# The second MLP's first product, taken for two token tiles at once as seven half-size products instead of eight

## The reference

```
h = x @ w_in                                  # (1536, 512) @ (512, 2048)
x2 = (h * 1/(1 + exp(-1.702 h))) @ w_out      # (1536, 2048) @ (2048, 512)
```

```
h = x2 @ w_in                                 # (1536, 512) @ (512, 1024)
e = exp(h - max(h)); sm = e / sum(e); solu = h * sm          # along a token's 1024 values
ln = (solu - mean) / sqrt(var + 1e-6) * g_ln
out = ln @ w_out                              # (1536, 1024) @ (1024, 512)
```

## Time and profile before

| | us |
|---|---|
| median of 3 runs | 672.72 (672.15 to 673.79) |
| profiled execution, its own time | 672.1 |
| its span, first to last instruction | 670.3 |
| PE busy | 639.0 (95%) |
| DVE busy | 434.5 (65%) |
| POOL busy | 419.7 (63%) |
| ACT busy | 321.0 (48%) |

### The profile page before, as it was taken

The page is one execution under the profiler, slowest core; times in us unless marked ns, Lnnn a source line. Parts: engine busy times, 40 slices in busy tenths (PEclk is TensorE's granted clock), DMA queues, the critical chain, the costliest instruction groups (busy, mean ns, idle before and its releaser), DMA issues.

```text
span 670.3 us, 11572 instructions
## 1 busy us (share of the span) xinstructions
PE 639.0 (95%) x3281; PEld 537.8 (80%) x3281; DVE 434.5 (65%) x759; ACT 321.0 (48%) x641; POOL 419.7 (63%) x590
## 2 busy tenths in 40 slices
PE   5689999999999999999999999999999999999998
PEld 1369989898989888788877888788888878888886
DVE  3779999999999985666657667562222554545352
ACT  1279999999999984222232222132222243324232
POOL 2677788798888886888878888878886100000000
PEclk9779999999999999999999999999999999999999
DMA  8866544544544421232222222222231022112101
GB/s 284 245 185 154 159 120 112 143 122 126 143 112 137 130 92 64 72 113 87 104 94 93 90 99 94 94 95 94 94 106 51 29 82 77 52 60 78 63 16 47
DMA packets 39601, 70.52 MB, mean 105 GB/s; under 512 B 4256, under 2 KB 22688, under 8 KB 39584
## 3 DMA queue, kind: packets, MB, share of 16 engines
q1 hardware_dynamic: 37568, 66.38, 33.1%
q10 hardware_dynamic: 2016, 3.93, 1.6%
HBM read 46.60 MB, written 4.72 MB: 77 GB/s over the span
## 4 chain that ended last, share of the span: by engine, by line
PE 68%; ACT 10%; issue 9%; DVE 5%; DMA 4%; POOL 2%; DVEq 1%; SPq 1%; ACTq 0%; POOLq 0%
PE banks L534 6%; PE banks L549 6%; PE banks L551 6%; PE banks L550 6%; PE banks L564 6%; PE banks L566 6%; PE banks L565 5%; PE banks L639 5%; ACT probs L761 4%; PE banks L519 4%; PE banks L672 3%; PE banks L671 3%; PE banks L670 3%; ACT probs_th L772 3%; PE banks L642 2%
## 5 line engine op out<-in xcount | busy, mean ns | idle before, releaser
L979 DVE TENSOR_TENSOR probs_tl<-banks,probs_th 128x384 fp32r<-128x384 f32 x192 | 100.5, 547 | 11.7 <-ACT probs_th L772 9.4
L959 DVE TENSOR_REDUCE neg_max<-banks 128x1 f32<-128x768 f32 x96 | 91.3, 951 | 8.6 <-PE banks L506 6.6
L772 ACT CAST probs_th<-banks 128x384 fp32r<-128x384 f32 x192 | 83.0, 485 | 20.8 <-PE banks L519 19.5
L761 ACT ACTIVATE probs<-banks,neg_max 128x768 f32<-128x768 f32 x96 | 88.3, 920 | 7.1 <-DVE neg_max L959 7.0
L953 DVE TENSOR_TENSOR gl<-gate,gh 128x512 fp32r<-128x512 f32 x48 | 48.2, 1003 | 66.8 <-ACT gh L746 66.8
L1145 POOL TENSOR_TENSOR wait_scrap<-half_power 128x1 f32<-128x1 f32 x176 | 46.4, 264 | 67.1 <-PE banks L566 33.7
L1221 POOL TENSOR_SCALAR probs<-probs,row_inv 128x768 f32<-128x768 f32 x96 | 87.0, 907 | 0.0
L1284 POOL TENSOR_TENSOR stat<-stat,half_power 128x1 f32<-128x1 f32 x12 | 6.6, 549 | 127.5 <-DVE stat L1092 127.5
L519 PE MATMUL banks<-ident,probs 128*128 128x128 f32 x576 | 79.0, 273 | 1.3 <-ACT hot_t L715 1.3
L534 PE MATMUL banks<-probs_th,v_parts 128*128 128x384 f32 x192 | 70.4, 367 | 9.8 <-DVE x_sums L986 9.8
L746 ACT CAST gh<-gate 128x512 fp32r<-128x512 f32 x48 | 29.8, 621 | 101.1 <-PE banks L566 52.7
(11 more groups left out here) (100 smaller groups left out, 1346.1 us busy)
## 6 DMA issues: line engine op xcount, KB each, us to landing
gelu_raw<-w_gelu SPq DMA_DIRECT2D x48, 512.0 KB, 3.3
ln_raw<-w_ln SPq DMA_DIRECT2D x8, 512.0 KB, 4.3
pair_t<-q_t SPq DMA_DIRECT2D x4, 768.0 KB, 7.3
pair_t<-k_t SPq DMA_DIRECT2D x4, 768.0 KB, 8.2
kq_raw<-k_t SPq DMA_DIRECT2D x16, 192.0 KB, 3.5
kq_raw<-q_t SPq DMA_DIRECT2D x16, 192.0 KB, 3.7
q_parts<-k_high SPq DMA_DIRECT2D x16, 192.0 KB, 2.6
q_high<-k_high SPq DMA_DIRECT2D x16, 192.0 KB, 3.0
```

The costliest lines, as they stand in the source:

```text
L761: nc.scalar.activation(probs[:, n % NP, :].rearrange("p (c t) -> p c t", c=2), scores[n % 2], ACT.Exp, bias=neg_max[:, n % NP:n % NP + 1], ...
L772: nc.scalar.copy(probs_th[half % 2][:, c * CH:(c + 1) * CH, i * P:(i + 1) * P], pt_bank(n, c).rearrange("p (t s) -> p t s", t=CH)).then_in ...
L959: nc.vector.tensor_reduce(out=neg_max[:, col], in_=scores[n % 2], op=ALU.max, axis=mybir.AxisListType.XY, negate=True).then_inc(max_done, 1)
L979: nc.vector.tensor_tensor(probs_tl[half % 2][at], pt_bank(n, c).rearrange("p (t s) -> p t s", t=CH), probs_th[half % 2][at].bitcast(F32), ...
```

## The change

Two token tiles (a pair) and the two halves of features and hidden units make a product of 2x2 blocks by 2x2 blocks. Before, it is formed as eight block products; after, as seven products of sums of blocks (Strassen's scheme in Winograd's form). One block product is 6 matmuls of 128x512, so a pair has 42 in place of 48.

- **Right operands.** Four sums of weight blocks (T1 to T4) are formed on DVE, and seven blocks are split. This stands in the first MLP's second block: 36 operations of 128x512 in 8 steps, where 8 `split_ln` (24 operations) stood. The first block keeps its 24.
- **Left operands.** Four sums (S1 to S4) and seven splits, 18 operations of 128x256 for each pair. For pair 0 DVE does them in the first MLP's third block; for pairs 1 to 5 POOL does them, each chain started by the end of the seven products of the pair before. The two root operations of that pair stand inside and behind this chain on POOL.
- **x2** is no longer split at the end of a block: ACT writes it once, DVE's `x2_low` and all `move_tile` DMAs go.
- **Results.** Each product fills one PSUM bank. ACT copies the first to SBUF, DVE forms the four result blocks by seven sums of 128x512 (u2, u4, u3, c11, c21, c22, c12). Maximum, exponential, solu, square and norm then read and write SBUF.
- **PE's order** is for a pair: seven products, turn2 of the pair before's tile 0, down2 of tile 1 of the pair two before, turn2 of tile 1, down2 of tile 0. Pair 1 differs: turn2(0,0) stands between its fourth and fifth product, and after its products only turn2(0,1) and down2(0,0) follow. All seven products of pair 0 stand ahead of `block_tail`. The loops are written out.

```diff
+            def product(it, i):
+                if it == 0:
+                    pe.wait_ge(lhs0_step, LHS_READY[i])
+                else:
+                    pe.wait_ge(lhs_step, (it - 1) * LHS_STEPS + LHS_READY[i])
...
+                if order == TWO:
+                    pe.wait_ge(one_copied, it + 1)
+                if order == FOUR:
+                    pe.wait_ge(u2_done, it + 1)
+                if order == THREE:
+                    pe.wait_ge(u3_done, it + 1)
+                dst = product_ps[i]
+                for k in range(HK):
+                    nc.tensor.matmul(dst, lhs_h[:, i, k, :], rhs_h[:, i, k, :], start=k == 0, stop=False)
+                    nc.tensor.matmul(dst, lhs_h[:, i, k, :], rhs_low(i, k), start=False, stop=False)
+                    last = nc.tensor.matmul(dst, lhs_l[:, i, k, :], rhs_h[:, i, k, :], start=False, stop=k == HK - 1)
+                last.then_inc(product_done, 1)
...
+            for it in range(1, PAIRS):
+                for i in range(PRODUCTS):
+                    if it == 1 and i + 1 == TWO:
+                        turn2(0, 0)
+                    product(it, i)
+                if it > 1:
+                    turn2(it - 1, 0)
+                    down2(it - 2, 1)
+                turn2(it - 1, 1)
+                down2(it - 1, 0)
+            turn2(PAIRS - 1, 0)
+            down2(PAIRS - 2, 1)
+            turn2(PAIRS - 1, 1)
+            down2(PAIRS - 1, 0)
+            down2(PAIRS - 1, 1)
```

The order on DVE, with the products in the order one, six, five, seven, two, four, three:

```diff
+            for it in range(PAIRS):
+                u2_sum(it)      # product six + the copy of product one
+                u4_sum(it)      # product five
+                u3_sum(it)      # product seven
+                if it == 1:
+                    lnt_low(0, 0)
+                c11_sum(it)     # product two
+                c21_sum(it)     # product four
+                c22_sum(it)
+                max_tile(it, 0)
+                c12_sum(it)     # product three
+                max_tile(it, 1)
+                solu_tile(it, 0)
+                if it > 1:
+                    lnt_low(it - 1, 0)
+                if it == 1:
+                    lnt_low(0, 1)
+                solu_tile(it, 1)
+                variance(it, 0)
+                norm_tile(it, 0)
+                variance(it, 1)
+                norm_tile(it, 1)
+                if it > 1:
+                    lnt_low(it - 1, 1)
```

The order on POOL:

```diff
+            for it in range(1, PAIRS):
+                pool.wait_ge(x2_done, KT + (it // (BL // (2 * P)) + 1) * KT)
+                pool.wait_ge(product_done, it * PRODUCTS)
+                lhs_split(it, 0, A11, x2_tile(it, 0, 0))
+                lhs_sum(it, 2, S1, x2_tile(it, 1, 0), x2_tile(it, 1, 1), ALU.add)
+                lhs_sum(it, 3, S2, lhs_exact(S1), x2_tile(it, 0, 0), ALU.subtract)
+                lhs_sum(it, 4, S4, x2_tile(it, 0, 1), lhs_exact(S2), ALU.subtract)
+                lhs_split(it, 5, S2, lhs_exact(S2))
+                lhs_split(it, 7, S1, lhs_exact(S1))
+                root(it - 1, 0)
+                lhs_sum(it, 9, S3, x2_tile(it, 0, 0), x2_tile(it, 1, 0), ALU.subtract)
+                lhs_split(it, 10, S3, lhs_exact(S3))
+                lhs_split(it, 12, A12, x2_tile(it, 0, 1))
+                lhs_split(it, 14, A22, x2_tile(it, 1, 1))
+                lhs_split(it, 16, S4, lhs_exact(S4))
+                root(it - 1, 1)
```

More of the change, by code:

```diff
@@ L409, in _ @@
                 gelu_turn(it)
[L412 to L432, removed]
             for u in range(2):
-                sp.wait_ge(out_stored[u], 16 * FREE + 16 * (TT // 2))
+                sp.wait_ge(out_stored[u], 16 * PAIRS)
         @block.tensor
@@ L625, in _ @@
             block_body(NBL - 1)
[L628 to L643, removed]
@@ L657, in turn2, with down2 @@
                     last = nc.tensor.transpose(lnt_ps[:, k // KT, k % KT * P:(k % KT + 1) * P],
-                                               normed[u][:, k * P:(k + 1) * P], ident[:])
+                                               hid[it % 2][u][:, k * P:(k + 1) * P], ident[:])
                 last.then_inc(turn2_done, 1)
-            def down2(it, u, start=0, end=F2 // P):
+            def down2(it, u):
                 t = it * 2 + u
                 n = F2 // P
[L664 to L694, removed]
+                pe.wait_ge(lnt_l_done, t + 1)
+                if it > 0:
+                    pe.wait_ge(out_copied[u], it)
+                for k in range(n):
+                    nc.tensor.matmul(out_ps[u], lnt_h[u][:, k, :], ln_h[:, k, :], start=k == 0, stop=False)
+                    nc.tensor.matmul(out_ps[u], lnt_h[u][:, k, :], down_low(k), start=False, stop=False)
+                    last = nc.tensor.matmul(out_ps[u], lnt_l[u][:, k, :], ln_h[:, k, :], start=False, stop=k == n - 1)
@@ L1035, in _, with lhs0_sum @@
+            def lhs0_sum(order, i, left, right, op):
+                dve.wait_ge(lhs0_step, order)
+                nc.vector.tensor_tensor(lhs_exact(i), left, right, op).then_inc(lhs0_step, 1)
             dve.wait_ge(gains_loaded, 16)
@@ new lines, in lhs_sum, with root @@
+            def lhs_sum(it, order, i, left, right, op):
+                pool.wait_ge(lhs_step, (it - 1) * LHS_STEPS + order)
+                nc.gpsimd.tensor_tensor(lhs_exact(i), left, right, op).then_inc(lhs_step, 1)
+            def root(it, u):
+                pool.wait_ge(var_done, it * 2 + u + 1)
+                nc.gpsimd.tensor_tensor(stat[:, u, 9:10], stat[:, u, 8:9], half_power[:], ALU.pow).then_inc(root_done, 1)
+            for it in range(1, PAIRS):
+                pool.wait_ge(x2_done, KT + (it // (BL // (2 * P)) + 1) * KT)
[13 more added lines that the diff above has]
+                root(it - 1, 1)
@@ L1288 @@
+            for u in range(2):
+                root(PAIRS - 1, u)
 def kernel(q, k, v, centroids, moe_w_in, moe_w_out, moe2_w_in, moe2_w_out, moe2_g_ln):
```

402 lines of the change are left out of this document (278 added, 124 removed).

## The result

The changed kernel takes 681.48 us (median of 4 runs, 679.80 to 683.09) where the kernel before takes 672.92 (672.15 to 673.79): a ratio of 1.0127 [1.0093, 1.0160], slower. In a later round the two stood at 682.84 and 672.95, 1.0140 [1.0092, 1.0187]. The first median lies 0.02 us inside the upper end of the range that the prediction gave (671.5 to 681.5), the second outside. The profiled execution took 682.8 us, its span is 681.0. Over the rounds the kernel before, unchanged, ran in 670.3 to 676.5 us.

A forecast was written before the change was run, and what follows sets the result against it. The second MLP was taken as bound by PE alone, 148.5 us; 138.4 us of work plus 15.0 of waits gave 153.4, 4.9 more, so 677.0 us on the profiled execution's 672.1; 8-in-10 range 671.5 to 681.5.

The forecast's parts named there:

- Product four's two waits: Second MLP: PE waits for DVE's sum u2 behind norm 1, 2.6 us in pair 1 and 3.5 in pair 2.
- POOL slower: Rival, chance 0.10: POOL 10% slower or DVE's one-element operations wait for it; pairs 3 to 5 lose cover; 679 to 681.5 us.
- the cases that end slower: Forecast case (675 to 679) 0.55, slower POOL 0.10, falling clock 0.03, stretched first MLP 0.02; slower was given as 0.68.
- matmuls and old waits: Second MLP on PE: 36 matmuls fewer, 8.2 us, and three old waits gone, 1.9 us; 10.1 us gained.
- new waits: Second MLP on PE: 2.4 + 2.6 + 3.1 + 3.5 + 1.9 + 1.5 = 15.0 us of waits added.
- Product seven: Second MLP: PE waits for POOL's sum and split of S3, 2.4 us in pair 1 and 3.1 in pair 2.
- Turns and drain: turn2 waits for lnt_low: tile 1's turns 0.5 us in each of four pairs, 1.9 in all; the drain's turn2(5,0) 1.5.
- Contention: Each solu, norm and scale on DVE waits for POOL's operation under way and POOL for them; without the lock 2.1 us less.
- The clock: Rival, chance 0.03: the clock falls in pairs 1 and 2, some 3 us of work in each taking twice as long; 683 us.
- costed at nothing: First MLP: added right-operand work on DVE fits beside POOL, 1.6 us free per 11.0; else up to 1 us in 8 steps.
- would move by no more than 0.5: Sign: the first MLP's end, at 518.6 us, should not move by more than 0.5 us.
- The rival of the stretched first MLP: Rival, chance 0.02: DVE and POOL stretch the first MLP in its second block, up to 8 us on top, 685 us.

The follow-up runs named there:

- the second profile: The changed kernel run once more with nothing edited: 682.84 us, 1.0140 of the kernel before; its second MLP takes 155.8 us.
- the one with earlier operands and the moved tile: Changed kernel with left operands started as buffers free, roots behind them, and the turned tile in the weight slices' place: 669.93 us, 0.9943 of the kernel before.
- the spread right operands: Changed kernel with the 36 right-operand operations spread over 14 DVE steps of the first MLP's second and third block: 681.62 us, 1.0128 of the kernel before.
- both edits: Changed kernel with earlier left operands, and u2, u4, u3 ahead of the previous tile's variance and norm for pairs 1 and 2: 676.20 us, 1.0031 of the kernel before.
- ACT's downh: Kernel with earlier left operands and the moved tile, plus ACT casting each down slice's high part instead of POOL: 684.88 us, 1.0177 of the kernel before.

## Why the prediction was right or wrong

Slower, as forecast, and in the second MLP by the mechanism forecast: what the product saves is lost to waits of the products for POOL's left operands and DVE's sums. Product four's two waits came out within 0.02 us. But the time is 4.5 us above 677.0, by errors in both directions, and outside the forecast's own 675 to 679: the loss was forecast as 4.3 us on the medians and measured as 8.6. That it fell inside the wider range, by 0.02 us, is luck; the rival whose stretch it fell into (POOL slower, 679 to 681.5) is not what happened, since its sign, waits of product four in pairs 3 to 5, didn't come. (The chances of the cases that end slower add up to 0.70, not to the 0.68 given.)

**The second MLP** (153.9 us, 153.4 predicted) agrees by cancelling. From the 148.5 of before:

| term | predicted | measured |
|---|---|---|
| matmuls and old waits | -10.1 | -9.5 |
| new waits | +15.0 | +10.5 |
| clock behind the waits | 0 | +1.4 (3.6 in the second profile) |
| down2 reads its tile at another place | 0 | +1.7 |
| not assigned | 0 | +1.2 |
| sum | +4.9 | +5.3 |

The old waits, taken like the new ones as distances of starts, were 1.3 us and not 1.9. The kernels with few waits leave a like rest (the one with earlier operands and the moved tile: 138.4 + 3.1 of waits = 141.5 against 142.9).

- *Product seven* was over-estimated (2.4 and 3.1 against 1.70 and 1.06). DVE and POOL in pair 2 of the kernel after show why, in order of time:
```profile
561.42 1.20 DVE L1247 TENSOR_TENSOR xh<-banks,xh 128x1024 fp32r<-128x1024 f32 x1
562.54 1.21 DVE L1233 CUSTOM_DVE_ANT_0 gelu_raw<-gelu_raw,exp 128x1024 f32<-128x1024 f32 x1
...
564.67 0.55 POOL L1469 TENSOR_TENSOR stat<-stat,half_power 128x1 f32<-128x1 f32 x1 [0.32 <-DVE stat L1258]
...
566.51 1.04 POOL L1460 TENSOR_TENSOR lhs_l<-lhs_sums,lhs_h 128x256 fp32r<-128x256 f32 x1
```
lnt_low (L1247) runs in the 0.9 us in which DVE would stand for the exp of tile 1 (0.92 idle at this point in pair 1); I had added it in full. The sums and the lnt_low ahead of the first max cost nothing either: that max starts with POOL's first step in both pairs. With POOL's first step at T1 = 556.27 the variance is out at T1 + 8.3, not + 10.2, and S3 is ready at T1 + 11.3, not + 13.4. In pair 1 all steps came 0.2 to 0.6 early (S3 at T0 + 11.2 for 11.8). Product four's waits came out right all the same because both sides of them count from S3: TensorE has two products to do, POOL and DVE the rest of the chain, the root, the norm and u2, and product four started 6.4 us after S3 in both pairs (6.3 forecast).
- *Turns and drain* were over-estimated too: 1.08 and 0.54 for 1.9 and 1.5. I put it down to the same reserve; no run tests it.
- *Contention* was rightly charged: solu and POOL's splits stretch each other.
- *The clock* was a rival with 0.03. Its evidence was thin both ways, and I counted the absence of such a wait in the trace as evidence against it. Of the seven profiles with a wait of over 2.4 us in the second MLP four show it: this rival deserved about even odds. Its price was too high: a fall cost 1.4 or 2.2 us, where some 3 in each of two pairs were taken.
- *down2's place* was never asked about: I took the new operand at the old cadence. This is a failed step, not a mis-sized one.

**The first MLP**: "costed at nothing" failed. The earlier trace rows have 1.6 us of POOL free in each 11.0, and I held the added DVE operations to less than that. What I left out is that they stretch POOL's own: upl went from 1318 to 1608 ns, a slice's POOL operations from 4.74 to 5.18 us. Little of it shows in the view of waits (0.3 us of PE); it shows in the starts of `up`'s first matmuls. The "would move by no more than 0.5" was the test for it, and it moved by 2.0 (5.4 with the first stage); PE's busy time fell by 2.6 us where about 8 was the sign. By its own signs the prediction is wrong on this stage. The rival of the stretched first MLP had a chance of 0.02 and up to 8 us; its mechanism was right at a quarter of its size.

**The first stage**: +3.4 us was forecast by nobody. The kernel after, in order of time:
```profile
24.72 0.55 PE L489 MATMUL banks<-ident,sims_t 128*128 128x128 f32 x3 [0.60 <-ACT sims_t L741]
29.57 1.50 PE L477 MATMUL banks<-pair_t,c_diag 128*32 128x384 f32 x8 [4.31 <-DMA pair_t<-k_t]
```
TensorE stood 4.31 us for this load of the third pair, 1.34 for the same one in the kernel before. The change doesn't touch it, and over eleven more profiles the first `up` stands at 250.1 to 256.3 us, so I take it for the scatter that also spreads the kernel before by 6 us. Their mean with the kernel after's is 252.7, and the kernel before has one profile (251.1), so a shift of about 1 us can't be excluded. Taken off the profile it leaves 7.3 us for the change; the medians differ by 8.6 and, in the later round, by 9.9, and the clock's fall, of varying length, would cover the difference. This last balance is argued, not shown.

## What to carry to other kernels

When work moves off the engine that is the bound, list what its operands need on the side engines between two uses, and start each piece at the release of its own buffer: here that, with the roots behind the chain, was worth 7.9 of the 10.5 us of waits, and with the tile moved it made a loss of 1.3% a gain of 0.6%. Follow each re-ordering to what is queued behind the moved instruction; two orders that each removed waits made new ones together. An operation costed at nothing because "the engine has room" is to be costed again by what it holds up meanwhile.

## What the runs showed of the hardware

- The granted clock fell to 0.50, for 2.5 to 5 us of work at a time (6 to 12 matmuls 0.43 us apart), after waits of 2.4 to 3.9 us in seven places (the kernel after once, the same again twice, the spread right operands and both edits once each, ACT's downh twice), and didn't after waits of 2.4, 2.6, 3.4 and 3.5 us in others. After the wait of 3.5 us in pair 2 the same kernel did both, in two executions.
- Back-to-back 128x512 matmuls of one shape went at 0.227 or 0.233 us depending on where in SBUF the weight-side tile lay: 21 steps took 4.85 or 4.98 us, of which the first, behind the turn, takes 0.31.
- POOL's 128x256 tensor_tensor takes 742 ns and its tensor_scalar 405 ns alone, and no longer beside DVE's max over SBUF or its lnt_low, which has one PSUM operand (738 and 405 ns at 561 to 563 us of the kernel after). Where one meets solu, of two SBUF operands, they take 1.6 and 1.26 us.
- Moving a 0.62 us copy from POOL to ACT lengthened the first MLP by 14.5 us, through a dependence between two in-order engines, not through load: POOL stood idle for 6.38 us for the copy.
